# Attention with decay and two feed-forward layers: where the last column of an attention unit is computed

## The reference

```
f = sigmoid(f_logit)
for t in range(S):
    state = f[t][:, None] * state + outer(k[t], v[t])
    y[t] = q[t] @ state
x  = y as (3072, 384)
x1 = elu(x @ w_in) @ w_out          # elu: h > 0 ? h : exp(h) - 1
out = (relu(x1 @ w_in2) ** 2) @ w_out2
```

## Time and profile before

| | us |
|---|---|
| median of 3 runs (lowest, highest) | 978.47 (978.26, 981.43) |
| the profiled execution's own time | 977.67 |
| its span in the trace | 975.9 |
| PE busy | 953.0 (98%) |
| PEld busy | 786.8 (81%) |
| DVE, ACT, POOL busy | 504.7, 402.1, 237.8 |

### The profile page before, as it was taken

The page is one execution under the profiler, slowest core; times in us unless marked ns, Lnnn a source line. Parts: engine busy times, 40 slices in busy tenths (PEclk is TensorE's granted clock), DMA queues, the critical chain, the costliest instruction groups (busy, mean ns, idle before and its releaser), DMA issues.

```text
span 975.9 us, 27520 instructions
## 1 busy us (share of the span) xinstructions
PE 953.0 (98%) x11636; PEld 786.8 (81%) x11636; DVE 504.7 (52%) x746; ACT 402.1 (41%) x706; POOL 237.8 (24%) x193
## 2 busy tenths in 40 slices
PE   7799989999999999999999999999999999999998
PEld 6677777888888788888878888888888888888897
DVE  7788576565757657563326663343343343433432
ACT  4555545344535443454444453242332422423322
POOL 3002215363635464454423641000000000000000
PEclk9999999999999999999999999999999999999999
DMA  7461422303130212212003331002020020020100
GB/s 240 152 195 41 127 67 68 99 2 100 36 97 24 79 65 69 65 48 68 1 2 109 97 86 66 1 8 58 1 50 14 0 61 3 7 57 0 19 15 33
DMA packets 72426, 56.87 MB, mean 58 GB/s; under 512 B 37248, under 2 KB 64640, under 8 KB 72320
## 3 DMA queue, kind: packets, MB, share of 16 engines
q1 hardware_dynamic: 69472, 43.87, 16.7%
q10 hardware_dynamic: 2848, 11.44, 3.3%
HBM read 45.84 MB, written 9.44 MB: 57 GB/s over the span
## 4 chain that ended last, share of the span: by engine, by line
PE 94%; DVE 2%; issue 2%; ACT 1%; DMA 1%; SPq 0%; DVEq 0%; ACTq 0%
PE ps L1669 8%; PE ps L1665 8%; PE ps L1664 8%; PE ps L1139 7%; PE ps L1688 7%; PE ps L1684 7%; PE ps L1685 7%; PE ps L1278 6%; PE ps L1301 6%; PE ps L1280 5%; PE ps L1287 5%; PE ps L1303 5%; PE ps L1307 5%; PE ps L1208 2%; PE ps L1156 1%
## 5 line engine op out<-in xcount | busy, mean ns | idle before, releaser
L1609 DVE TENSOR_TENSOR g<-g 128x512 f32<-128x512 f32 x96 | 66.8, 696 | 240.9 <-ACT g L1524 240.3
L1524 ACT ACTIVATE g<-ps 128x512 f32<-128x512 f32 x112 | 67.0, 598 | 276.9 <-PE ps L1669 272.6
L694 POOL TENSOR_TENSOR glo<-g,ghi 128x512 fp32r<-128x512 f32 x65 | 89.7, 1379 | 194.0 <-ACT ghi L519 194.0
L1664 PE MATMUL ps<-xhi,wts 128*128 128x512 f32 x336 | 130.9, 390 | 0.0
L1665 PE MATMUL ps<-xhi,wts 128*128 128x512 f32 x336 | 130.9, 390 | 0.0
L878 DVE SCALAR_TENSOR_TENSOR g<-e,g 128x512 f32<-128x512 f32 x80 | 57.9, 724 | 140.3 <-ACT g L513 140.3
L512 ACT ACTIVATE e<-ps 128x512 f32<-128x512 f32 x80 | 47.9, 598 | 162.6 <-PE ps L1287 162.6
L1684 PE MATMUL ps<-ghi,wts 128*128 128x512 f32 x294 | 114.4, 389 | 0.0
L1685 PE MATMUL ps<-ghi,wts 128*128 128x512 f32 x294 | 114.4, 389 | 0.0
L1278 PE MATMUL ps<-xhi,wts 128*128 128x512 f32 x240 | 98.9, 412 | 0.2 <-ACT g L513 0.2
L1669 PE MATMUL ps<-xlo,wts 128*128 128x512 f32 x336 | 94.6, 390 | 0.0
(11 more groups left out here) (132 smaller groups left out, 1559.4 us busy)
## 6 DMA issues: line engine op xcount, KB each, us to landing
raw<-w SPq DMA_DIRECT2D x52, 192.0 KB, 2.4
q<-qk SPq DMA_DIRECT2D x22, 256.0 KB, 5.0
gate<-fl SPq DMA_DIRECT2D x10, 512.0 KB, 5.5
k<-qk SPq DMA_DIRECT2D x10, 512.0 KB, 3.7
x<-xo ACTq DMA_DIRECT2D x6, 768.0 KB, 3.3
xs<-x ACTq DMA_DIRECT2D x6, 768.0 KB, 4.4
v<-vn SPq DMA_DIRECT2D x11, 384.0 KB, 4.0
krow<-vn SPq DMA_DIRECT2D x20, 192.0 KB, 4.5
```

What stands on the lines that cost most here:

```text
L694: nc.gpsimd.tensor_tensor(out=glo[:, f % 2, :], in0=g[:, f % 2, :], in1=ghi[:, f % 2, :].bitcast(F32), op=ALU.subtract).then_inc(s_glo, 1)
L1664: nc.tensor.matmul(h, w(0, k), xhi[:, k, :], start=(k == 0), stop=False)
```

## The change

From unit 4's period on, TensorE's order is another one:

- group 1: last column of unit n-1 (from unit 5 on), (n, 4); slots 15 of the period before, 0, 1
- group 2: (n, 5), (n+1, 0); slots 2, 3, 4
- group 3: (n, 6), (n+1, 1); slots 5, 6, 7
- group 4: (n+1, 2), transposed keys; slots 8, 9, 10
- group 5: q_state part 0, (n+1, 3), q_state part 1, values of both halves, new_state; slots 11 to 14

The last unit keeps q_state, new_state and q_state together, followed by both halves of values, and has its last column between slots 13 and 14. The special code for unit 3 gives up its slot 15, so that its last column and (4, 4) stand side by side. The other engines' programs are put in the matching order, levels 0 and 1 alone go to the Y pair from unit 5 on, and some waits name another event:

```diff
@@ level_pair
+        if past(c, h, 5):
+            return pair(c, h, "Y" if l < 2 else "A")
@@ ACT: acc_copy in three parts
-            nc.scalar.activation(xo[:, :, :], ps[:, ACC:ACC + KD, :], ACT.Copy).then_inc(s_acc, 1)
+            for m in range(KD):
+                done = nc.scalar.activation(xo[:, m, :], ps[:, ACC + m, :], ACT.Copy)
+                done.then_inc(s_acc if m == KD - 1 else s_accs, 1)
@@ ACT: period
+            if past(c, h, 5):
+                y_copy(*unit_before(c, h))
             hidden_copies(c, f - 1)
@@ DVE: period
+            step(c, h, 4)
             activate(c, f - 1)
             if h == 0:
                 x_split(c)
...
+            if more(c, h):
+                take(c, h + 1, 3)
+                q_update(c, h + 1, 3)
+                double(c, h + 1, 3)
             state_update(c, h)
@@ PE: product
-            elif l in (1, 2):
+            elif l == (2 if past(c, h, 5) else 3):
+                pe.wait_ge(s_ev6, count(c, h, 1, 0))
+            elif l in (1, 2, 3):
                 pe.wait_ge(*taken(c, h, l))
-            elif l == 3:
-                pe.wait_ge(s_ev6, count(c, h, 1, 0))
@@ PE: q_state, part 1
+            elif past(c, h, 4) and more(c, h):
+                pe.wait_ge(*level(s_mm, c, h + 1, 3))
@@ PE: output
-            if f == 0 and begun(c, 0, 1):
-                pe.wait_ge(s_acc, c - 1)
             start, stop = n == NF, n == 2 * NF - 1
             for m in range(KD):
+                if f == 0 and begun(c, 0, 1):
+                    pe.wait_ge(*((s_acc, c - 1) if m == KD - 1 else (s_accs, (c - 2) * (KD - 1) + (m + 1))))
@@ PE: period
-            for i in range(3):
-                group(c, h, i)
-                feed(c, h, range(3 * i, 3 * i + 3))
-            end_of_levels(c, h)
-            feed(c, h, (9, 10))
-            y_and_state(c, h)
-            feed(c, h, (11, 12))
-            end_of_y(c, h)
-            feed(c, h, (13, 14, 15))
+            if past(c, h, 5):
+                last_column(*unit_before(c, h))
+            product(c, h, 4)
+            feed(*unit_before(c, h), (15,))
+            feed(c, h, (0, 1))
+            product(c, h, 5)
+            if more(c, h):
+                product(c, h + 1, 0)
+            feed(c, h, (2, 3, 4))
+            product(c, h, 6)
+            if more(c, h):
+                product(c, h + 1, 1)
+            feed(c, h, (5, 6, 7))
+            if more(c, h):
+                product(c, h + 1, 2)
+            transpose_keys(c, h)
+            feed(c, h, (8, 9, 10))
+            if more(c, h):
+                q_state(c, h, 0)
+                product(c, h + 1, 3)
+                q_state(c, h, 1)
+                values(c, h, 0)
+                values(c, h, 1)
+                new_state(c, h)
+                feed(c, h, (11, 12, 13, 14))
+            else:
+                y_and_state(c, h)
+                values(c, h, 1)
+                feed(c, h, (11, 12, 13))
+                last_column(c, h)
+                feed(c, h, (14, 15))
@@ PE: second_period
-            feed(1, 1, (15,))
```

More of the change, by code:

```diff
@@ L156, in attention @@
     s_o, s_acc, s_x2 = sem("output_products"), sem("acc_copied"), sem("x2_stored")
+    s_accs = sem("first_acc_blocks_copied")
     s_xhi, s_xlo = sem("xhi_ready"), sem("xlo_ready")
@@ L284, in more, with unit_before @@
         return 2 * c + h + n < UNITS
+    def unit_before(c, h):
+        return divmod(2 * c + h - 1, 2)
     @blk.sync
@@ L540, in period @@
             hidden_copies(c, f)
+            take5(c, h)
+            high(c, f)
             if h == 0:
                 acc_copy(c)
-            high(c, f)
             hidden_copies(c, f + 1)
-            take5(c, h)
             if h == 0:
@@ L548, in period @@
             high(c, f + 1)
+            pad_v(c, h)
+            take6(c, h)
             hidden_copies(c, f + 2)
             high(c, f + 2)
-            pad_v(c, h)
-            take6(c, h)
             hidden_copies(c, f + 3)
@@ L561, in period @@
             high(c, f + 5)
-            y_copy(c, h)
             hidden_copies(c, f + 6)
+            if not more(c, h):
+                y_copy(c, h)
             high(c, f + 6)
@@ L708, in period @@
             f = 8 * h
+            k_update(c, h, 4)
             low(c, f - 1)
-            k_update(c, h, 4)
             if more(c, h):
                 keep_last(c, h + 1)
+            k_update(c, h, 5)
+            low(c, f)
+            if more(c, h):
                 k_update(c, h + 1, 0)
-            low(c, f)
-            k_update(c, h, 5)
+            low(c, f + 1)
+            k_update(c, h, 6)
             if more(c, h):
                 k_update(c, h + 1, 1)
-            low(c, f + 1)
             low(c, f + 2)
-            k_update(c, h, 6)
+            low(c, f + 3)
             if more(c, h):
                 k_update(c, h + 1, 2)
-            low(c, f + 3)
+            low(c, f + 4)
             if more(c, h):
                 k_update(c, h + 1, 3)
-            low(c, f + 4)
             decay_state(c, h)
@@ L904, in period @@
                 x_split(c)
[L905 to L912, removed]
             activate(c, f)
@@ L915, in period @@
             if more(c, h):
-                step(c, h + 1, 1)
+                take(c, h + 1, 0)
+                q_update(c, h + 1, 0)
+                double(c, h + 1, 0)
             activate(c, f + 1)
-            activate(c, f + 2)
             step(c, h, 6)
             if more(c, h):
-                step(c, h + 1, 2)
+                step(c, h + 1, 1)
+            activate(c, f + 2)
             activate(c, f + 3)
@@ L926, in period @@
             if more(c, h):
-                step(c, h + 1, 3)
+                step(c, h + 1, 2)
             activate(c, f + 4)
@@ L1149, in transpose_keys @@
             elif more(c, h):
-                pe.wait_ge(*taken(c, h + 1, EARLY - 1))
+                pe.wait_ge(*taken(c, h + 1, 2 if past(c, h, 4) else EARLY - 1))
             else:
```

## The result

| | before | after |
|---|---|---|
| median (lowest, highest), us | 979.22 (978.26, 981.43), 4 runs | 994.03 (993.11, 995.78), 4 runs |
| profiled execution, us | 977.67 | 993.52 |
| its span, us | 975.9 | 991.7 |
| PE busy, us | 953.0 | 956.8 |

The change makes the kernel slower by a factor of 1.0149 (95% interval 1.0128 to 1.0169). Forecast were +8.2 us on the profiled execution; measured are +14.8 between the medians and +15.8 between the spans.

A forecast was written before the change was run, and what follows sets the result against it. TensorE's matmul stream was taken to bound the kernel, with instruction fetch interrupting it. Terms -3.3 + 0.8 + 9.1 + 1.9 - 0.3 = +8.2 us on 977.67 gave 985.9; forecast median 986.5, range 977 to 990.

The forecast's parts named there:

- (g): Fifth groups of units 4 to 10: 288 matmuls outrun instruction fetch, TensorE stands 0.8 to 1.5 us; +9.1 us.
- (h): Unit 4's merged group of 176 matmuls: block edge comes earlier, packet does not; +1.9 us, down to 0.
- rival C: Something besides: transfers collide, `new_state` waits for DVE, or the clock falls after (h)'s gap; 991 to 997 us, chance 0.07.
- (c): Tile starts of units 4, 6, 8, 10: one big step covers `x_split`, hidden step 0.2 us longer; +0.8 us.
- (a): Units 4 to 11: 40 groups instead of 48, each saving 0.26 us; 2.1 us saved.
- (b): Last column no longer waits 0.22 us for the values before it, eight times; saves 1.8 us less about 0.6.
- (i): The existing 0.3 us gap at 319.78 goes into (g); -0.3 us.
- (d): Fifth group: `new_state` waits for DVE to take level 3; 0, up to +0.7 us a period.
- (e): `acc_copy` has one step of cover instead of a step and a group; 0, up to +0.2 us four times.
- A: Rival: instruction fetching keeps up, so the change is faster; 976.0 or 974.4 us, chance 0.15.
- D: Rival: DVE, not fetch, bounds the fifth group; 980.9 us, chance 0.02.
- B: Rival: packets follow edges at the quick end, 0.8 us a period, and (h) costs nothing; 981.3 us, chance 0.08.

The follow-up runs named there:

- e9: Kernel before with values of half 1 moved beside half 0, so its fifth group has 224 matmuls; 985.9 us, ratio 1.0059.
- e4: Kernel after with 16 unneeded matmuls ahead of values in units 4 to 10; 1000.4 us, ratio 1.0204.
- e8: Kernel after with the fifth group cut in two by two slots and DVE's activate ahead of state_update; 991.8 us, ratio 1.0101.
- e15: Kernel after with unit 5's loads of v and staged v held until unit 5's level 0; 993.9 us, ratio 1.0125.
- e6: Kernel after with POOL's low at a tile's start waiting for DVE's third x_split subtraction; 991.4 us, ratio 1.0118.
- e3: Kernel after with the edits of e1, e8 and e6 together; 986.0 us, ratio 1.0051.
- e12: Kernel after with the loads of unit 6's gates and what follows them held until unit 5's level 0 is done; 993.6 us, ratio 1.0140.
- e2: Kernel after with the fifth group cut into 128 and 160 matmuls, two slots between, DVE's order unchanged; 996.7 us, ratio 1.0176.
- e1: Kernel after with unit 3's slot 15 back between its last column and product 4 of unit 4; 994.2 us, ratio 1.0163.

## Why the prediction was wrong

The sign and the main mechanism were right: fewer, denser groups run TensorE out of instructions. The size was off by 6.5 us (8.2 against 14.7 behind the start; the start's own 1.2 us is scatter between profiles), and the range ended at 990.

| step | predicted | measured |
|---|---|---|
| (g) seven fifth groups | +9.1 | +8.4 (0.74, 1.73, 0.82, 1.31, 0.99, 0.83, 1.96) |
| (h) gap at the border | +1.9 | +1.8 (3.14 against 1.35) |
| clock behind it | in rival C alone | +1.65 |
| unit 11's group | none | +1.67 |
| (c) tile starts | +0.8 | +2.5 |
| (a), (b), (i) savings | -3.6 | -1.3 (what is left of the sum) |
| (d), (e), (f) | 0 | 0 seen |
| sum | +8.2 | +14.7 |

- **(g)** held in size, place and mechanism. e9, e4 and e8 show the mechanism from three sides: add density and gaps come, add time and they close, cut the group and most go. The count of 193 in 256 puts every gap at a block's edge. It missed one case of its own rule: unit 11's group (`q_state`, `new_state`, `q_state`, both values) was not counted, and its block ended one matmul into the next `hidden`, 1.67 us at 514.54.
- **(h)** held in size, and e15 shows its cause. But the step ended there: a gap of 3.1 us sets the clock to half. That was in rival C, with the 3.5 us named; it got 0.07 because no row that I had read had such a gap at full clock. The trace of the kernel before has one. Behind an "issue" gap of 2.58 us, at a clock of 1.00 until then, the clock was 0.50 from 43.91 us on, for 3.4 us (timeline of PE and window, columns PE, clock, DMA share, GB/s):

```profile
43.34 0.98 PE L1228 MATMUL ps<-PT,vz 64*64 64x64 f32 x48 [2.58 <-issue]
...
43.90:47.30 3.40, 3.40 (x104) 0.50 0.02 5
```

The prediction speaks of three "issue" gaps; the trace of before holds seven, and this is the longest. Read next to the 1.35 us at which the clock stayed, it spoke for putting the 1.7 us into the sum. One part of C thus came true on top of the forecast, and C's range (991 to 997) held the time.
- **(c)** failed. I took the one tile start with this order in the trace, where POOL had nothing to do beside the subtractions, as standing for four. Units 4, 8 and 10 cost some 0.1 to 0.3 more than a bare step; unit 6 cost 1.7, because POOL's `low` began 0.13 us ahead of DVE's third subtraction. In the other three it began 0.24 us behind it, and the subtraction took its 0.68. e6 shows it.
- **(a), (b)** failed. With gaps, waits and half clock taken off, the part behind unit 3's last column is as long as before (828.8 and 828.5 us), and the periods take 45.3 to 45.6 us against 45.3 to 45.6. Groups were counted, but not their pieces. A product that stands alone takes more: level 3 takes 1.12 us to the next instruction (184.92 to 186.04) where it took 0.96, and two products that stood together took 0.87 each where alone they take 0.85 to 1.1. The small matmuls of a period take 11.4 us before and 11.4 to 11.6 after, though the drain of (b) is gone, which saved 0.2 us a period in e9. The big steps take 34.0 us before and 33.8 after where no tile starts.
- **The failed steps in one line.** The clock behind (h), left to rival C, measured 1.65 to 1.7 us; unit 11's group, left out of (g), 1.67; (c) was 1.7 too small, for the collision of POOL and DVE; and the savings (a) and (b) were 2.3 too large.
- **Rivals.** A (no fetch stall) and D (DVE as the bound) are excluded by e4 and e8. B (0.8 us a period) was the bottom end of the gaps measured.

The Trainium skill, "Runtime: NRT & Kernel Launch", section "Instruction fetch mechanics", has blocks of 256 instructions and the cost of an edge mostly hidden. The trace agrees on the size. It agrees on hidden only where a block lasts longer than the 2.9 to 3.9 us from edge to next block: most edges show no gap, and those of the kernel after show one at which a block is used up in 1.8 to 2.3 us. The 128 KiB that it gives for TensorE is neither shown nor refuted. In the trace of before no q8 packet comes between 683.28 and 906.40 us, while 986 matmuls pass with their weight loads. There TensorE repeats the loop over the tiles, three times without a packet, and an iteration has 288 matmuls and 288 weight loads. So more than two blocks stay in store. What the gaps exclude is that the blocks ahead are already there: in a plain stream the next one is asked for one block ahead. The step of the prediction from eight blocks in store to no gap does not hold for that reason.

Left open: why the time from packet to usable block differs between profiles, from 2.2 to 3.0 us (it makes unit 5's gap 1.73 us in one and 2.23 in another; their packets came 1.1 us behind the edge in both); why the packet of the 1.83 us gap comes 5.0 us behind its edge; and why that gap had half clock behind it in e8 and none in e3.

## What to carry to other kernels

Count instructions a microsecond, not only microseconds: where small matmuls use up a block of 256 instructions (here 128 matmuls with their weight loads) in less than the 3 us that the next one needs, break a group up by large matmuls. Joining groups here lost 0.7 to 2 us a period where 0.26 a group was hoped for, and no net saving came of it. Look for idle time that ends with "issue" and count to it: the same remainder each time is a block's edge. Price the second effect of every gap that you accept: what the clock does behind it, and which loads run while the block is asked for. When work moves to other cover, look at each place where it lands for what the other engines do at that moment, not at one that stands for all.

## What was not expected of the hardware

- The granted clock was 0.50 for 3.4 us behind every gap of 3.0 to 3.4 us (after, e4, e6, e8, e9, e12), and for 6.8 us at the one of 4.1 us (e2), from 1.2 us before its end. Behind gaps of 1.2 to 2.2 us it came in some profiles (1.18 and 1.83 us in e8, 2.23 and 1.97 in e15) and not in others (1.96 in after, 1.84 in e3, 1.18 in e1). Each stretch of 3.4 us cost about 1.7.
- The packet of an instruction block waits for the load traffic: at unit 3's end 2.3 to 3.3 us behind the edge at a DMA share of 0.6 to 1.1 up to the packet, 0.8 us at 0.04.
- TensorE repeats a loop body of 288 matmuls and 288 weight loads, more than two blocks, without a packet (710.0 to 905.8 us in before), and yet stands at the edge of a block in a plain stream.
- A subtraction of 128x512 on DVE takes 0.69 us alone and 1.77 when one of POOL began 0.13 us before it (unit 6's tile).
- The last column in blocks of 64 and 32 columns instead of 32 takes 1.01 us instead of 0.51, though it has fewer instructions.
